# Weighted sums of blocks 4 to 8: one burst of TensorE a pair of heads in place of two

## The reference, cut to what matters

```python
# stage 1: attention, 4 batches x 8 heads, 576 rows of 64; 9 blocks of 64 rows, masked by blocks
scores = scale * np.matmul(q, k.transpose(0, 1, 3, 2))
scores = np.where(block_i >= block_j, scores, -1e9)
attn = np.exp(scores - max); attn = attn / (sum + 1e-9)
x = np.matmul(attn, v)                # [4, 8, 576, 64] -> [2304, 512]
# stage 2: dense layer
h = x @ w_in; x = (h - np.tanh(h)) @ w_out
# stage 3: routed layer, 8 experts, each token to one of them or passed through
out[do_compute] = xc + gate_w * (np.maximum(xc @ w1[e], 0.0) @ w2[e])
```

## Time and profile before

| | before |
|---|---|
| median of three runs | 899.11 us (898.79 to 899.45) |
| the profiled execution, own time | 903.3 us |
| its span, first to last instruction | 901.0 us |
| mean granted TensorE clock | 0.967 of full speed |
| TensorE busy | 838.6 us, 93% of the span |
| VectorE / ScalarE / GpSimd busy | 478.8 / 328.9 / 258.2 us |
| attention | from the start to about 196.5 us |

### The profile page before, as it was taken

How to read it: one execution, slowest core, us unless ns; L and a number is a source line. 1 busy time by engine, 2 the same in 40 slices (tenths; PEclk the granted TensorE clock), 3 DMA queues, 4 the chain that set the end, 5 groups by cost and what they waited for, 6 DMA issues and landing times.

```text
span 901.0 us, 18923 instructions
## 1 busy us (share of the span) xinstructions
PE 838.6 (93%) x6038; PEld 719.0 (80%) x6039; DVE 478.8 (53%) x1224; ACT 328.9 (37%) x852; POOL 258.2 (29%) x329
## 2 busy tenths in 40 slices
PE   5999999979999999999999999999549779999993
PEld 3555555549999999999999999999537658888882
DVE  5788888865553443544444444443634566556161
ACT  4677777741121211212212122221504555545260
POOL 4777777768301010010100101001123312333331
PEclk9999999999999999999999999999769989999998
DMA  8244444313100000000000000007033655665100
GB/s 173 62 103 104 102 103 104 77 45 115 37 7 22 0 26 0 10 16 0 26 0 17 9 0 26 1 27 188 27 117 107 210 196 190 217 206 197 64 23 8
DMA packets 83193, 66.77 MB, mean 74 GB/s; under 512 B 63162, under 2 KB 63162, under 8 KB 83152
## 3 DMA queue, kind: packets, MB, share of 16 engines
q1 hardware_dynamic: 77824, 60.56, 23.5%
q0 software_dynamic: 4144, 5.38, 1.8%
q10 hardware_dynamic: 1184, 0.30, 0.2%
HBM read 60.86 MB, written 9.08 MB: 78 GB/s over the span
## 4 chain that ended last, share of the span: by engine, by line
PE 91%; DVE 2%; DMA 2%; issue 1%; ACT 1%; POOL 1%; ACTq 0%; POOLq 0%; DVEq 0%; SPq 0%
PE psum L1100 66%; PE psum L1030 6%; PE psum L1008 6%; PE psum L979 5%; PE psum L964 2%; PE psum L1136 2%; PE psum L1211 1%; PE psum L1144 1%; PE psum L1188 1%; ACT we L552 1%; DVE neg_max L729 1%; DMA q_rows<-in_q_dram 1%; DVE x_lo L777 0%; DMA xg<-out_dram,rec_next 0%; POOL probs L455 0%
## 5 line engine op out<-in xcount | busy, mean ns | idle before, releaser
L644 ACT ACTIVATE tanh_h<-psum 128x288 f32<-128x288 f32 x128 | 52.5, 410 | 313.4 <-PE psum L1100 299.4
L1100 PE MATMUL psum<-x_hi,wi_hi 128*128 128x288 f32 x512 | 155.0, 303 | 2.9 <-ACT x_hi L552 1.6
L1100 PE MATMUL psum<-x_lo,wi_hi 128*128 128x288 f32 x512 | 152.3, 297 | 0.0
L1100 PE MATMUL psum<-x_hi,wi_lo 128*128 128x288 f32 x512 | 151.9, 297 | 0.0
L1100 PE MATMUL psum<-g_hi,wo_hi 128*128 128x288 f32 x512 | 150.8, 295 | 0.0
L1100 PE MATMUL psum<-g_hi,wo_lo 128*128 128x288 f32 x512 | 150.7, 294 | 0.0
L1100 PE MATMUL psum<-g_lo,wo_hi 128*128 128x288 f32 x512 | 150.6, 294 | 0.0
L845 DVE TENSOR_TENSOR g<-psum,tanh_h 128x288 f32<-128x288 f32 x128 | 58.5, 457 | 146.4 <-ACT tanh_h L644 142.1
L479 POOL DMA_INDIRECT lists<-rec,slot_i x24 | 23.6, 983 | 368.6 <-DVE slot_i L834 318.3
L455 POOL TENSOR_SCALAR probs<-probs,row_inv 128x384 f32<-128x384 f32 (+2 forms) x96 | 97.7, 1027 | 59.0 <-DVE row_inv L736 59.0
L1100 PEld LDWEIGHTS psum<-x_hi,wi_hi 128*128 128x128 f32 x512 | 97.2, 190 | 3.9 <-issue 3.9
(11 more groups left out here) (136 smaller groups left out, 1332.5 us busy)
## 6 DMA issues: line engine op xcount, KB each, us to landing
w_half<-in_moe_w_dram SPq DMA_DIRECT2D x64, 512.0 KB
q_rows<-in_q_dram SPq DMA_DIRECT2D x32, 144.0 KB, 3.0
out_dram<-x_rows SPq DMA_DIRECT2D x24, 192.0 KB, 2.1
k_rows<-in_k_dram SPq DMA_DIRECT2D x30, 144.0 KB, 3.2
v_rows<-in_v_dram SPq DMA_DIRECT2D x32, 128.0 KB, 2.3
w_raw<-in_moe_w_in_dram SPq DMA_DIRECT2D x16, 256.0 KB, 3.5
w_raw<-in_moe_w_out_dram SPq DMA_DIRECT2D x16, 256.0 KB, 2.5
v_rows<-in_v_dram SPq DMA_DIRECT2D x32, 16.0 KB, 2.2
```

What stands on the lines that cost most here:

```text
L644: act.activation(tanh_h[:, f % 2, :], h_ps[:, f % 2, 0:CH], ACT.Tanh).then_inc(tanh_done, 1)
L1100: mm = pe.matmul(dst, w, m, start=(first and n == 0), stop=(last and n == 2), skip_group_check=True)
```

## The change

The two calls of `weigh_many` for a pair are put together where the second stood: all five chunks are summed in one burst behind the second part of the keys and queries, in front of the turns of step 0. No instruction is added and none is removed; the tail for pair 15, behind the loop, keeps its two calls.

```diff
@@ -1069,7 +1069,6 @@
                     turn_keys(u + 1, 0)
                     turn_queries(u + 1, 0)
                 if u > 0:
-                    weigh_many(u - 1, (0, 1))
                     turn_first(u - 1, 3)
                     turn_second(u - 1, 3)
                 score(u, 2)
@@ -1077,7 +1076,7 @@
                     turn_keys(u + 1, 1)
                     turn_queries(u + 1, 1)
                 if u > 0:
-                    weigh_many(u - 1, (2, 3, 4))
+                    weigh_many(u - 1, (0, 1, 2, 3, 4))
                 turn_first(u, 0)
                 turn_second(u, 0)
                 score(u, 3)
```

## The result

| | before | after |
|---|---|---|
| median (6 runs each) | 898.95 us | 906.8 us |
| span of the profiled execution | 901.0 us | 908.3 us |
| TensorE busy | 838.6 us (93%) | 837.9 us (92%) |
| scores of pair 1 to scores of pair 15 | 158.72 us | 165.95 us |

The ratio on record is 1.0069, with a 95% interval from 1.0048 to 1.0090: slower by 4.3 to 8.1 us. The two medians of the table lie 7.9 us apart, inside this interval and near its upper end. Forecast were 6.7 us and 905.8, in a range from 903.2 to 909.0.

What follows compares the result with a forecast made beforehand. TensorE's sequence at full clock was taken to pace each pair. 0.51 us in 13 pairs (6.63), plus 0.28 for pair 1, less 0.22 for pair 15, gave 6.7 on 899.1: 905.8 us, range 903.2 to 909.0.

Steps and rivals of the forecast that it cites:

- rival D: The stall is taken back elsewhere and nothing measurable is left: about 899.5 us, chance 0.03.
- Point 1: Turns of step 3, without the first burst as cover, wait for ScalarE's copy of the keys: 0.68 us stall, 0.55 earlier start.
- Point 2: Score step 2 and second keys, coming 0.55 us earlier, find their inputs ready: cost nothing, with 0.3 us of thin cover.
- Point 4: Joined burst in front of the turns of step 0: its inputs are older than before when it asks; ScalarE's queue keeps its place.
- Point 3: Chunks 0 and 1 inserted before chunks 2 to 4 cost 1.06 us for 1.23; burst edges paid once save 0.17.
- Rival A: Stall without the joint's saving, edges belonging to each chunk or the restart costing as much: 9.3 us, 908.4 us, chance 0.13.
- Points 5 and 6: Pairs at the ends of the loop: pair 1 loses 0.28 us (late queries' copy), pair 15 gains 0.22 (no keys and queries).
- Rival C: Clock behind attention shifts: 902.5 us if its cost of about 3.3 falls away, 909.1 if as much is added; chance 0.06.
- rows 9: Profile rows behind attention, read as TensorE idling most of 5 us, then running at 0.50 clock, costing about 3.3 us.
- rival B: Copies don't hold the turns of step 3, only the joint's saving is left: -0.17 us in 15 pairs, 896.5 us, chance 0.04.

Runs made afterwards that it cites:

- the control: Kernel before, with VectorE alone reordered to copy the turns of step 3 before taking the reciprocals of step 0: ratio 1.0064, pair 11.85 us.
- the second measurement: The changed kernel unaltered, run again beside new runs of the kernel before: 909.4 against 901.8 us, ratio 1.0078.

## Why the prediction was right

**What bounds the pair: right.** TensorE's sequence, at full clock. The stall of 0.68 us that was forecast, of which 0.61 is on record as idle time, less the joint's 0.15, is the 0.53 by which a pair grew; nothing else made up for it. That also answers rival D, in which the stall was to be taken back elsewhere.

**Point 1, the cover: right to the hundredth.** Turns 0.05 us behind the copy, at 4.40 into the pair (forecast 92.69 - 88.30 = 4.39), the second turn 0.27 behind and free of its own wait. The copy sooner, the copy with its cover halved, and the turns in other banks each did what this reading asks.

**Point 2, no second wait: right.** None for `pt` in front of the keys: the copy of the turns ends at 96.57 and the second keys start at 96.98, so the slack is 0.4 us where 0.3 was read. Point 4 holds too: no wait stands in front of the joined burst in pairs 1 to 15.

**Point 3, the joint: right in kind, the sum 0.02 too good.** I took an insertion of 1.06 (0.17 saved). Measured are 2.35 us for 2.50, 0.15 saved, which makes the pair 0.53 longer, not 0.51. The bound that I named and left, an edge as large again, is there (12.13 - 11.83 = 0.30 for the whole). But in the change it lies at the first burst's old place, in front of the wait, and is hidden by it; point 3 had looked for it at the seam in front of the second burst and did not see this. The rule that a change of tiling mode drains TensorE (the Trainium skill, TensorEngine Tiling (Array Packing), section Key Properties) agrees with the runs here as far as they go: 0.30 us for entering and leaving 128x64 once more. Rival A is refuted: an edge for each chunk by the same run, and a restart as dear as the saving by the change itself, whose pair (11.83) has the 0.15 in it.

**Points 5 and 6: right in the sum.** From pair 1 to pair 15 it is 7.23 us (forecast 6.63 + 0.28 = 6.91). Thirteen times the missing 0.02 is most of the difference, and pair 1 alone grew by 0.34. Pair 15, up to its turns of step 0, took 193.03 - 185.66 = 7.37 in place of 186.30 - 178.72 = 7.58: 0.21 sooner, forecast 0.22. Together 7.0 us, against 6.2 measured by the ratio (4.3 to 8.1), 7.9 between the medians, or 7.6 between those of the second measurement. Since single executions of the change lie 4 to 6 us apart, it is in part luck that the median came within 1.0 us of 905.8; what bears the forecast out is the pair, 0.53 longer for 0.51.

**Rival C was a condition, not an alternative.** The mean clock differs between executions of one kernel, before (0.965 at 903.5 us, 0.970 at 898.9) and after alike (0.965 at 910.0, 0.972 at 905.7); where it differs is shown for the change only. It widens what is measured by some 2 to 3 us each way and decides nothing on the sign. The reading of rows 9 also said that TensorE idles for most of 5 us in front of the lower clock; it is busy for 2.62 us from 195 to 200. I had given it a chance of 0.06 as another outcome; it belonged in the width of every outcome.

**The drain rule alone (rival B)** has the right sign for the joint: the kernel with own banks is faster than before. But its condition, that the copies don't hold the turns, is false (the wait of 0.61): the change as made takes away a cover of which 0.68 us was needed, to save 0.3 of edges, of which it sees half.

## What to carry to other kernels

Work that stands between a producer and the next user of the same bank is a cover, even when no wait is on record there: before moving it, read when the bank's copy ends and how much cover that needs (here 0.68 us, and 0.69 was enough). Joining two bursts of one tiling mode was worth 0.3 us a pair here (0.17 when the burst between scores and turns was joined too), and becomes a gain once the seam that is laid bare uses other banks. A queue without waits on the bounding engine does not make other engines' order free: one copy asked for too early on VectorE, in the kernel before, cost 0.55 us a pair.

## What the runs showed of the hardware that I had not expected

- A burst in 128x64 between transposes costs 0.30 us beyond its passes. Beside the kernel before, the run with own banks and VectorE's sooner copy shows where it lies. The joined burst takes 2.36 us from start to start (81.96 to 84.32), where the two took 2.50: 0.14. From the first queries to the work behind them it is 0.33 (79.61 to 79.94) for 0.43 (91.58 to 92.01), 0.10 in front of the burst's first pass. The first of the turns behind it take 0.23 for 0.27 (0.04). The stretch from which I read 0.17 holds only the first of these three parts.
- VectorE's scaling of 320 columns (L741) takes 0.39 us, but 1.17 to 1.28 us where it starts beside GpSimd's split of the weights (L448, a TENSOR_TENSOR of 1.27 to 1.28 us). The rows of the control and of the run with own banks, in which VectorE's order is that of the kernel before:

```profile
100.36 1.28 DVE L741 TENSOR_SCALAR probs<-probs,row_inv 128x320 f32<-128x320 f32 x1
```

```profile
83.41 1.17 DVE L750 TENSOR_SCALAR probs<-probs,row_inv 128x320 f32<-128x320 f32 x1
```

  In the twelve profiles 88 of these scalings start during the split, one of them in pair 0 of the kernel before (1.18 us). Each ends 0.17 to 0.19 us behind the split, whether it started 0.17 or 0.28 us after it. The other 104 take 0.39 to 0.41, most of them beside GpSimd's own scaling (L455). So, as far as 192 cases show, it is held up by that one instruction of GpSimd, which itself does not get longer. The Trainium skill (GPSIMD Engine Reference, section Specifications) says that GpSimd's interfaces to SBUF are shared with VectorE and that some of VectorE's instructions contend with it, which agrees with these rows.
- Executions of one kernel differ by up to 6 us. In the two profiles of the change, which have the same length of pairs, the clock in the last sums of attention and at the end of the dense stage makes 3.6 of 5.2 us. What sets the clock's place there was not tried.
